# Router logits inside the attention in fp32, smaller array tiles for scores and state product, state decay on ScalarE

## What is computed

```python
for t in range(768):                       # B=4, H=8, S=768, D=48
    cur = einsum('bhd,bhe->bhde', u * k[t], v[t])
    y[t] = einsum('bhd,bhde->bhe', r[t], state + cur)
    state = w * state + einsum('bhd,bhe->bhde', k[t], v[t])
x = y, transposed to [3072, 384]           # 8 heads x 48 side by side
# layer 1: rows with x @ w_skip > 0 only
e = argmax(x @ w_gate); g = softmax(x @ w_gate)[e]
x[row] += g * (relu(x[row] @ w1[e]) @ w2[e])     # E=8, 384 -> 1024 -> 384
# layer 2: every row
e = argmax(x @ w_gate2); g = softmax(x @ w_gate2)[e]
out[row] = g * (relu(x[row] @ w1b[e]) @ w2b[e])
```

## Time and profile before

| what | us |
|---|---|
| median of 3 runs | 663.84 (663.01 to 665.62) |
| profiled execution, its time | 663.71 |
| span in its profile | 662.0 |
| attention, start to end | 0 to 153.5 |
| first routing | 153.5 to 188.0 |
| first expert stage | 188.0 to 353.5 |
| second routing | 353.5 to 400.5 |
| second expert stage | 400.5 to 662.0 |

### The profile page before, as it was taken

One profiled execution on the slowest core, in us unless ns is written; L12 is line 12 of the kernel. 1 busy time (PEld: TensorE's weight loads), 2 busy tenths in 40 slices (PEclk: granted clock), 3 DMA queues, 4 the chain that ended last, 5 costly groups with the idle time before them and its releaser, 6 DMA issues. The chain is left out here.

```text
span 662.0 us, 15907 instructions
## 1 busy us (share of the span) xinstructions
PE 604.8 (91%) x5337; PEld 578.3 (87%) x5338; DVE 444.8 (67%) x854; ACT 229.9 (35%) x535; POOL 343.1 (52%) x413
## 2 busy tenths in 40 slices
PE   3999999997779998999974988999999999999994
PEld 3899999993669997999974687999999999999994
DVE  6899999993836876677771682756467583837432
ACT  1000000005106664555541602553346252626321
POOL 4998888863045665666660014444354362525321
PEclk9999999997999999999996999999999999999998
DMA  9677777766413557677614901527071643011100
GB/s 145 107 144 143 140 140 142 142 239 251 143 30 118 163 177 227 222 220 222 205 24 150 330 4 48 174 81 232 29 238 33 235 133 131 21 48 38 56 16 22
DMA packets 113724, 88.73 MB, mean 134 GB/s; under 512 B 80475, under 2 KB 104724, under 8 KB 113680
## 3 DMA queue, kind: packets, MB, share of 16 engines
q1 hardware_dynamic: 106304, 74.16, 39.8%
q0 software_dynamic: 7376, 14.03, 8.0%
HBM read 79.06 MB, written 13.57 MB: 140 GB/s over the span
## 5 line engine op out<-in xcount | busy, mean ns | idle before, releaser
L993 PE MATMUL e_ps_y<-w_lo,xT_hi 128*128 128x384 f32 x344 | 115.5, 336 | 0.0
L754 DVE TENSOR_TENSOR w_lo<-w_raw,w_hi 128x384 fp32r<-128x384 f32 (+1 forms) x80 | 69.1, 887 | 9.2 <-ACT w_hi L749 8.7
L908 POOL DMA_INDIRECT rows<-x_rows,e_ent_in x47 | 51.1, 1088 | 39.6 <-POOL e_ent_in L904 39.6
L1075 ACT CAST e_x_hi<-e_ps_x 128x384 fp32r<-128x384 f32 x47 | 22.6, 480 | 127.2 <-PE e_ps_x L978 120.6
L993 PEld LDWEIGHTS e_ps_y<-w_lo,xT_hi 128*128 128x128 f32 x344 | 64.8, 188 | 0.0
L992 PE MATMUL e_ps_y<-xT_lo,xT_hi 128*128 128x384 f32 x176 | 61.6, 350 | 0.3 <-DVE xT_hi L1179 0.3
L992 PE MATMUL e_ps_y<-w_hi,xT_hi 128*128 128x384 f32 x168 | 58.9, 350 | 0.7 <-DVE xT_hi L1179 0.6
L994 PE MATMUL e_ps_y<-xT_lo,xT_hi 128*128 128x384 f32 x176 | 59.4, 338 | 0.0
L749 ACT CAST w_hi<-w_raw 128x384 fp32r<-128x384 f32 (+1 forms) x112 | 57.5, 558 | 0.4 <-issue 0.2
L749 ACT CAST xT_lo<-w_raw 128x384 fp32r<-128x384 f32 (+1 forms) x112 | 57.4, 555 | 0.5 <-issue 0.2
L994 PE MATMUL e_ps_y<-w_hi,xT_hi 128*128 128x384 f32 x168 | 56.5, 336 | 0.0
(11 more groups left out here) (191 smaller groups left out, 1846.5 us busy)
## 6 DMA issues: line engine op xcount, KB each, us to landing
w_raw<-in_moe_w_dram SPq DMA_DIRECT2D x32, 1536.0 KB
r_in<-in_r_dram SPq DMA_DIRECT2D x24, 192.0 KB, 3.2
k_in<-in_k_dram SPq DMA_DIRECT2D x24, 192.0 KB, 3.9
v_in<-in_v_dram SPq DMA_DIRECT2D x24, 192.0 KB, 3.9
x_rows<-rows SPq DMA_DIRECT2D x24, 192.0 KB, 3.6
w_lo<-x_rows SPq DMA_DIRECT2D x4, 768.0 KB, 6.8
m_placing<-x_rows SPq DMA_DIRECT2D x2, 768.0 KB, 8.0
rows<-x_rows,e_ent_in POOLq DMA_INDIRECT x47
```

The costliest lines, as they stand in the source:

```text
L754: eng.tensor_tensor(self._of(self.lo1[par], self.lo2[par], n), self._of(self.raw1[par], self.raw2[par], n), self._of(self.hi1[par], self.h ...
L908: pool.indirect_dma_start(dst[:], None, rows, bass.IndirectOffsetOnAxis(ap=entry[:, 0:1], axis=0), bounds_check=bound, oob_is_err=False).t ...
L993: pe.matmul(o, s_hi, m_lo, start=False, stop=False)
L1075: act.copy(x_hi[:, :, SLOT[slot]], ps_x[:, 0:D].rearrange("p (c t) -> p c t", c=DC)).then_inc(x_hi_done, 1)
```

## The change

- In attention, `scores` use quarters of the array: the stationary operand is 64 rows by 64 columns, so a pair of heads takes four matmuls with 128 moving columns (16 for the step, formerly 8 on the whole array). Even heads go to one bank and odd heads to the other, and both are announced together. The zero padded copies of k are gone; k is scaled by one VectorE instruction instead of two.
- The state product is cut in two column halves (8 matmuls instead of 4) and moved ahead of the scores.
- The state update loads 48 columns of weights in place of 64, and `k_end` is 384 wide instead of 512.
- The decayed state is made by four ScalarE multiplications of 128x96 instead of one by GpSimd.
- ScalarE copies the transposed rows in fp32 to a small `xT`. Two steps later TensorE multiplies them with all 17 gate columns (`logits`, 3 fp32 matmuls on the whole array), and ScalarE copies the 17 columns to `lg`. VectorE's `xT_lo` is gone. At the end of the attention stand `logits`, `turn_x`, `logits` in a row.
- SyncE issues four weight loads instead of two ahead of the last four stores; the other two stood in the first routing.
- The first routing has no logit products. ScalarE's 14 high parts stand ahead of its Exp; GpSimd makes the 6 low parts of w1; VectorE makes the 8 low parts of w2 at the very end of its list.
- The second routing multiplies each transposed tile of 128 rows in fp32 with the 8 gate columns (3 matmuls for a tile) instead of four products per 512 rows.
- `xT_hi` and `xT_lo` are gone; the weight halves have SBUF of their own, and so has `hidden`.

```diff
@@ attention, SyncE
-            for matrix in range(2):
-                W.load(sp, matrix, 0, 0, 0)
+            for par in range(2):
+                for matrix in range(2):
+                    W.load(sp, matrix, 0, par, par)
             for sub in range(STEPS - B, STEPS):
                 store(0, sub)
@@ attention, GpSimd
-                pool.tensor_tensor(k_end[n][:], k_in[b][:], k_weight[:], ALU.mult).then_inc(k_end_done, 1)
-
-                wait(pool, state_done, i - 1)
-                pool.tensor_tensor(state_w[n][:], state[b][:].rearrange("p n (j d) -> p n j d", j=2),
-                                   w_pow[:, 7, :].unsqueeze(2).unsqueeze(3).to_broadcast([P, NP, 2, D]), ALU.mult).then_inc(decayed, 1)
+                pool.tensor_tensor(k_end[n][:], k_in[b][:, :, 0:D], k_weight[:, :, 0:D], ALU.mult).then_inc(k_end_done, 1)
@@ attention, ScalarE
-            def x_high(i):
+            def x_out(i):
 
                 wait(act, x_turned, i + 1)
-                act.copy(xT_hi[:, :, bass.ds(P * i, P)], ps_x[:, 0:HD].rearrange("p (c t) -> p c t", c=HD // P)).then_inc(xT_hi_out, 1)
+                act.copy(xT[:], ps_x[:, 0:HD].rearrange("p (c t) -> p c t", c=CH)).then_inc(xT_out, 1)
+
+            def logits_out(i):
+
+                wait(act, l_ready, i + 1)
+                act.copy(lg[:, bass.ds(i, 1), :].rearrange("p o g -> p (o g)"), ps_x[:, HD:HD + G]).then_inc(l_out, 1)
+
+            def decay(c, sub):
+                i, b, n = 4 * c + sub, sub % 4, sub % 2
+
+                wait(act, state_done, i - 1)
+                for p in range(NP):
+                    ins = act.mul(state_w[n][:, p, :, :].rearrange("p j d -> p (j d)"), state[b][:, p, :], w_pow[:, 7, p:p + 1])
+                ins.then_inc(decayed, 1)
...
             def step(c, sub):
                 i = 4 * c + sub
+                decay(c, sub)
+                if not (isinstance(i, int) and i < 2):
+                    logits_out(i - 2)
                 if not (isinstance(i, int) and i == 0):
-                    x_high(i - 1)
+                    x_out(i - 1)
@@ attention, VectorE
-                for j in range(2):
-                    q = slice(PAD * j, PAD * j + PAD)
-                    dve.tensor_tensor(k_sc[n][q, j::2, :], ps_k[q], shrink[q], ALU.mult).then_inc(scaled, 1)
+                dve.tensor_tensor(k_sc[n][:], ps_k[:], shrink[:], ALU.mult).then_inc(scaled, 1)
...
-                if not (isinstance(i, int) and i < 2):
-                    x_low(i - 2)
@@ attention, TensorE
             def turn_x(c, sub):
...
-                wait(pe, xT_lo_out, i)
+                wait(pe, l_out, i)
...
+            def logits(i):
+
+                wait(pe, xT_out, i + 1)
+                for m in range(CH):
+                    ins = pe.matmul(ps_x[:, HD:HD + G], xT[:, m, :], w_g[:, m, :], start=(m == 0), stop=(m == CH - 1))
+                ins.then_inc(l_ready, 1)
...
                 for p in range(NP):
-                    pe.matmul(ps_y[n][:, 2 * p:2 * p + 2, :].rearrange("p j d -> p (j d)"), r_sc[n][:, p, :], state[b][:, p, :], start=(p == 0), stop=False, skip_group_check=True)
+                    for t in (slice(0, P // 2), slice(P // 2, P)):
+                        pe.matmul(ps_y[n][t, 2 * p:2 * p + 2, :].rearrange("p j d -> p (j d)"), r_sc[n][:, p, t], state[b][:, p, :], start=(p == 0), stop=False, skip_group_check=True)
+
+                for p in range(NP):
+                    for t in (slice(0, P // 2), slice(P // 2, P)):
+                        for g in range(2):
+                            q = slice(PAD * g, PAD * g + PAD)
+                            ins = pe.matmul(ps_a[g][t, p, :], k_sc[n][q, p, t], r_sc[n][q, p, :], start=True, stop=True)
+                ins.then_inc(scored, 1)
...
+            logits(STEPS - 2)
             turn_x(0, STEPS - 1)
+            logits(STEPS - 1)
@@ routing, ScalarE
-            for g in range(TILES // GRP):
-                if g + 1 < TILES // GRP:
-                    xT_high(act, g + 1)
-                if not TURN:
-
-                    for n in range(2):
-                        W.hi(act, 0, 0, 2 * g + n)
-                act.wait_ge(lT_ready, g + 1)
...
+            else:
+                for n in range(W.N):
                     W.hi(act, 0, 0, n)
             act.wait_ge(z_ready, 1)
             act.activation(ez[:], z[:], ACT.Exp).then_inc(exp_done, 1)
@@ routing, VectorE, after the table
             dve.tensor_copy(table[:, :, 1].bitcast(F32), ps_table[:, 1, :]).then_inc(table_done, 1)
+            if not TURN:
+                for n in range(W.N1, W.N):
+                    W.lo(dve, 0, 0, n)
```

More of the change, by code:

```diff
@@ L69, in attention @@
         state_w = [sb(f"state_w{n}", [P, NP, 2, D]) for n in range(2)]
-        k_end = [sb(f"k_end{n}", [P, H, PAD]) for n in range(2)]
+        k_end = [sb(f"k_end{n}", [P, H, D]) for n in range(2)]
         ru = sb("ru", [P, H, D])
@@ L395, in route @@
     GP = TILES // PLACES
-    CH = xT_hi.shape[1]
-    E = w_gate.shape[1]
-    SK = 1 if w_skip is not None else 0
-    G = E + SK
+    CH = w_g.shape[1]
+    E = W.E
+    SK = 1 - m
+    COL = SK + E * m + m
     GRP = 512 // P
-    TURN = x_rows is not None
+    TURN = m == 1
     with ExitStack() as ctx:
@@ L451, in route @@
         if TURN:
+            turned_x = [sb(f"turned_x{n}", [P, CH * P]) for n in range(4)]
             spare = W.lo2[1][:].bitcast(F32)
@@ L505, in _ @@
             load_rows(sp)
-            if not TURN:
-                for k in range(2):
-                    W.load(sp, k, 0, 1, 1)
             for k in range(2):
@@ L533, in _ @@
             if not TURN:
-                for n in W.pool_pieces:
+                for n in range(W.N1):
                     W.lo(pool, 0, 0, n)
@@ L562, in _, with logits_of @@
+            def logits_of(i):
+                pe.wait_ge(xT_out, i + 1)
+                if i % GRP == 0 and i >= 2 * GRP:
+                    pe.wait_ge(l_out, i // GRP - 1)
+                for c in range(CH):
+                    ins = pe.matmul(ps_l[i // GRP % 2][:, i % GRP, :], turned_x[i % XT][:, P * c:P * c + P], w_g[:, c, COL:COL + E], start=(c == 0), stop=(c == CH - 1))
+                if i % GRP == GRP - 1:
+                    ins.then_inc(l_ready, 1)
             if TURN:
                 stay_warm(pe, ident, ps_xT[0][:, 0:P], 2)
-                turn_x(0)
@@ L583, in _ @@
-            turn(pe, TILES // GRP - 1)
+                for i in range(TILES + 2):
+                    if i < TILES:
+                        turn_x(i)
+                    if i >= 2:
+                        logits_of(i - 2)
             stay_warm(pe, ident, ps_xT[0][:, 0:P], 4)
@@ L760, in wait_split, with moe @@
         eng.wait_ge(self.lo_done[k][par], (self.N1, self.N - self.N1)[k] * (pair + 1))
-def moe(nc, m, W, rows, out_rows, ident, xT_hi, table, starts, x_in, y_row):
+def moe(nc, m, W, rows, out_rows, ident, hidden, table, starts, x_in, y_row):
     tag = f"e{m}"
@@ L791, in moe @@
         h_row = sb("h_row", [P, F])
[L793 removed]
+        h_hi, h_lo = [hidden[:, n, :].rearrange("p (k t) -> p k t", k=FC) for n in range(2)]
         ent_in = sb("ent_in", [P, 2], I32)
@@ L1256, in network @@
[L1256 to L1261 removed]
+            sp.dma_start(w_g[:, :, 0:1], w_skip.rearrange("(c p o) -> p c o", p=P, o=1), allow_slow_non_contiguous=True).then_inc(gates_loaded, 16)
@@ L1265 @@
+        route(nc, 0, W, None, ident, w_g, lg, hot, table, starts, order, stored)
+        moe(nc, 0, W, x_rows, x_rows, ident, hidden, table, starts, x_in, y_row)
+        route(nc, 1, W, x_rows, ident, w_g, lg, hot, table, starts, order, stored)
+        moe(nc, 1, W, x_rows, out, ident, hidden, table, starts, x_in, y_row)
 _INS = ["r", "k", "v", "w", "u", "moe_w_skip", "moe_w_gate", "moe_w1", "moe_w2", "moe2_w_gate", "moe2_w1", "moe2_w2"]
```

186 lines of the change are left out of this document (71 added, 115 removed).

## The result

The median of four executions is 685.68 us (685.13 to 690.23), against 663.42 (659.52 to 665.62) for the kernel before: a ratio of 1.036, 95% interval 1.030 to 1.041. The forecast was 672.4 in a range of 658 to 684. The direction was right, the size was not: 22 us slower instead of 8.6, and outside the range.

The account below looks back on a forecast made before the run. TensorE was taken to set the attention loop's pace, and a chain both routings. Terms of -1 (loop), +10 (attention's end), -6.6 and +2 (first routing) and +4.2 (second) gave +8.6 on 663.8: 672.4 us, range 658 to 684.

Parts of the forecast that it names:

- the half clock: Second routing: the first transposes run at half clock, costing +1.7 us within a stage term of +4.2.
- The product of counts: Second routing: three transposes and six records per tile take 0.99 us, for 24 tiles 23.9 us.
- The store's wait: End of the attention: a row store waits behind four weight loads instead of two, +8.0 us.
- The +2 for a low clock there: End of the attention: after idling, TensorE runs its chain at half clock, taken as +2 us.
- The attention step: Attention loop: savings and added costs sum to -0.05 us a step, -1 us in 23 steps.
- A change of shape at 0.16: Attention step: three more array shape changes at 0.16 us each add 0.48 us.
- The rival of the row halves: Attention scores: row halves take turns, scores stay at 1.78 us, total 693 us; chance 0.13.
- cheap logits: Attention and second routing: few moving columns make six records take 0.36 us, total 658 us; chance 0.10.
- free changes of shape: Attention step: shape changes among small tiles cost nothing, -11 us, total 661.4 us; chance 0.09.
- The first routing: First routing stage: -6.6 us for its chain and +2 for half clock and a load beside the first gather.
- the Exp behind the casts: First routing: `m_den` waits for the Exp behind 14 casts, starting after 7.6 us instead of 3.3, +4.3 us.

Follow-up runs that it names:

- e1_wide128: The changed kernel with the second routing's 8 gate columns padded with zeros to 128 moving columns: 662.59 us, ratio 0.999.
- e7_exp_first: The edits of e1_wide128 and e4_loads_after together, plus ScalarE's Exp ahead of its 14 weight casts in the first routing: 655.68 us, ratio 0.988.
- e4_loads_after: The changed kernel with the second expert's weight loads moved behind the last four row stores on SyncE: 676.11 us, ratio 1.019.
- e9_order: The edits of e1_wide128 and e4_loads_after together, plus attention steps reordered to three array shape changes instead of five: 652.55 us, ratio 0.985.
- e5_rows_in_turn: The changed kernel with the score matmuls reordered, all even heads first and then all odd heads: 695.76 us, ratio 1.049.
- e10_whole_scores: The edits of e1_wide128 and e4_loads_after together, but scores on the whole array with zero-padded k, as before the change: 682.91 us, ratio 1.033.
- e8_pool_late: e7_exp_first with GpSimd's six low parts moved behind its placing products in the first routing: 656.35 us, ratio 0.991.
- e3_warm_start: The changed kernel with 40 instead of 16 `stay_warm` transposes ahead of the second routing's loop: 682.0 us, ratio 1.028.

## Why the prediction was wrong, and where it was right

**The step that failed is the clock in the second routing.** The forecast took from the earlier trace rows that the half clock would cost 1.7 us at the start, as before, and then be over; before it was, with 24 transposes in a row there and matmuls of 512 columns from 364.63 on. In the changed kernel nothing but transposes and matmuls of 8 columns stands there, and the clock stayed at 1.2 GHz for 47.8 us, the last 5.1 of them under `stay_warm`'s transposes. The product of counts was right: tiles took 0.99 to 1.00 us in `e1_wide128`, with the clock, and `e7_exp_first`, whose loop starts on the half clock and then gets the full one, takes 26.0 us from the first transpose to the maximum (351.26 to 377.23), for 26.1 forecast. In this kernel the term should have been +24. With it the sum gives 692, and with the 4 us more that the loop gained, 688, between the median and the profiled execution. The missed question is what the busy time consists of. The forecast looked for idle time and found none. The Trainium skill supports that reading: TensorE: Matmul & The Clock Gate, Part 1, section What's actually happening, has the clock's ratio follow from how busy the engine has been recently, half by default and full when busy. Here TensorE was busy 37.00 of 37.00 us at 0.50, so the trace speaks against "busy" in the sense of a full queue; the same instructions with 128 columns ran at 1.00.

**The store's wait** was right: 9.0 us forecast as 8, the stage's end +10.1 as +10, and `e4_loads_after` took 9.3 us of it away. The +2 for a low clock there was of the right size: TensorE's work behind the wait lasted 2.3 us longer on 0.50.

**The attention step** was right in its parts: scores 1.03 (1.05), state product 0.82 (0.84), update 0.36, and the step 5.40 (5.48). A change of shape at 0.16 came out in `e9_order`, where two fewer gave 0.33. The rival of the row halves (693 us) falls with the 1.03 and with `e5_rows_in_turn` and `e10_whole_scores`, cheap logits with their 0.77 us in the step, and free changes of shape with `e9_order`. The loop gained 5.2 instead of 1 for two reasons. The forecast's own step was 0.08 long. And it took 5.53 from one step, while from step 4 on they average 5.56 before and 5.40 after, 3.2 us over 20 of them. The other 2.0 come before that: TensorE's first weight load stands at 8.11 for 9.07, and 1.0 comes in the first steps, two of which have no logits. I hadn't counted either, and what brought the earlier start is open.

**The first routing** came out at -5.3 for -4.6. Its total was right for a partly wrong reason. `m_den` did start after 7.8 us, but the Exp behind the casts accounts for 0.8 of it and VectorE's own instructions, drawn out beside GpSimd, for most of the rest (`m_den` comes after 3.3 us in `e8_pool_late`). The forecast hadn't priced GpSimd's low parts at all, because GpSimd isn't the limit of the stage.

## What to carry to other kernels

Before counting a stretch of TensorE at 2.4 GHz, look at what is in it, not only whether it is full: if wide matmuls leave it and matmuls of a few moving columns between transposes remain, find a row of the trace where such a mixture ran at the full clock, or put the half clock in the range. A matmul padded with zero columns can be cheaper than a narrow one. And count a load moved ahead of a store as a wait for everyone who needs that store's buffer.

## What the runs showed of the hardware

- The granted clock fell from 1.00 to 0.50 on a TensorE that was busy 6.80 of 6.80 us before and 41.00 of 41.00 after (`e3_warm_start`), with 8 moving columns between the transposes. With 32 it was 0.50 for 44.4 us, with 128 it was 1.00, and there it also rose from 0.50 in the loop (`e7_exp_first`).
- The 32 transposes of `stay_warm` did bring it back in the changed kernel (0.50 to 408.4, then 1.00, with nothing else on TensorE since 403.34), so the transposes alone don't hold it down. What separates the mixtures isn't settled by three widths.
- Matmuls on four quarters of the array: 32 records in 0.86 us when row halves alternate, 1.35 when they don't; on the whole array 16 records take 1.86 (`e10_whole_scores`).
- Between two groups of other array shape the weight loads pause 0.13 us (halves to quarters) and 0.17 (quarters to whole, whole to halves at the state product), but only 0.03 from the logits to the update and 0.05 from the scores times v to the transposes. Two changes fewer in a step gave 0.33 us.
- A VectorE instruction on 128x24 elements took 0.18 us alone and 1.15 beside GpSimd's two-input work (`e8_pool_late`, `e7_exp_first`).
